# Exp and state update named at earlier steps of a software-pipelined retention, SoLU and cosine-MLP kernel

## The reference

```python
# retention over 4 batches, 8 heads, 768 positions, head size 64
state = gamma * state + k_t^T v_t          # 64 x 64 per head
y_t   = q_t @ state / 8
x     = y as (3072 tokens, 512)
# SoLU block, 512 -> 1024 -> 512
h    = x @ w_in
e    = exp(h - max(h));  sm = e / (sum(e) + 1e-9)
solu = h * sm
ln   = (solu - mean) / sqrt(var + 1e-6) * g_ln
x2   = ln @ w_out
# cosine block, 512 -> 2048 -> 512
h = x2 @ w_in2;  out = (h * cos(h)) @ w_out2
```

## Time and profile before

| | |
|---|---|
| median of 3 runs | 966.66 us |
| the profiled execution, device time | 966.66 us |
| its span, first to last instruction | 964.9 us |
| PE busy | 933.9 us (97%) |
| DVE busy | 732.9 us (76%) |
| ACT busy | 562.7 us (58%) |
| POOL busy | 266.0 us (28%) |
| DVE slices of 24 us up to 384 us | all 70% or more, most 90% or more |
| granted TensorE clock, whole span | 0.986 |

### The profile page before, as it was taken

One profiled execution on the slowest core, in us unless ns is written; L12 is line 12 of the kernel. 1 busy time (PEld: TensorE's weight loads), 2 busy tenths in 40 slices (PEclk: granted clock), 3 DMA queues, 4 the chain that ended last, 5 costly groups with the idle time before them and its releaser, 6 DMA issues.

```text
span 964.9 us, 14709 instructions
## 1 busy us (share of the span) xinstructions
PE 933.9 (97%) x4992; PEld 831.1 (86%) x4992; DVE 732.9 (76%) x1054; ACT 562.7 (58%) x922; POOL 266.0 (28%) x260
## 2 busy tenths in 40 slices
PE   3899999999999999999799999999999999999998
PEld 3688888888888888888699999999999999999997
DVE  7989899989999899976556677656775666765564
ACT  5656657657566566554555566546665556656453
POOL 2465576666665765731000000000000000000000
PEclk8799999999999999999899999999999999999999
DMA  7413454634653535435796544744345544364401
GB/s 276 153 66 115 147 204 137 217 110 145 221 178 132 193 137 189 154 98 164 280 316 194 141 117 123 230 139 120 111 129 179 180 110 129 111 192 114 117 12 65
DMA packets 106520, 148.18 MB, mean 154 GB/s; under 512 B 7408, under 2 KB 77040, under 8 KB 106480
## 3 DMA queue, kind: packets, MB, share of 16 engines
q1 hardware_dynamic: 106480, 147.69, 47.6%
HBM read 112.01 MB, written 35.65 MB: 153 GB/s over the span
## 4 chain that ended last, share of the span: by engine, by line
PE 79%; DVE 13%; issue 5%; ACT 2%; DMA 1%; POOL 0%; DVEq 0%; SPq 0%; ACTq 0%; POOLq 0%
PE bank L310 26%; PE bank L312 26%; PE bank L313 26%; DVE p_l L1065 2%; DVE q_l L1049 1%; PE bank L596 1%; DVE work L1115 1%; DVE p_m L1058 1%; DVE nmax L1109 1%; DVE x_l L1089 1%; DVE wo_out L1158 1%; DVE z_l L1142 1%; ACT x_h L749 1%; PE bank L619 1%; DVE work L1150 1%
## 5 line engine op out<-in xcount | busy, mean ns | idle before, releaser
L310 PE MATMUL bank<-yc_h,ring 128*128 128x384 f32 x448 | 152.3, 340 | 5.8 <-ACT e L872 2.5
L312 PE MATMUL bank<-yc_l,ring 128*128 128x384 f32 x448 | 152.2, 340 | 0.0
L313 PE MATMUL bank<-yc_h,ring 128*128 128x384 f32 x448 | 151.7, 339 | 0.0
L1185 DVE SCALAR_TENSOR_TENSOR gg<-turns,c 128x768 f32<-128x768 int32 x64 | 61.0, 953 | 65.2 <-ACT turns L816 65.2
L989 POOL TENSOR_TENSOR y_raw<-y_raw,t 128x768 f32<-128x768 f32 x4 | 7.4, 1854 | 367.9 <-DVE yc_l L1167 367.8
L816 ACT ACTIVATE turns<-c 128x768 int32<-128x768 f32 x64 | 54.2, 846 | 81.0 <-DVE c L1255 78.2
L822 ACT ACTIVATE gg<-gg 128x768 f32<-128x768 f32 x64 | 54.2, 847 | 80.0 <-DVE gg L1192 79.9
L310 PEld LDWEIGHTS bank<-yc_h,ring 128*128 128x128 f32 x448 | 84.7, 189 | 14.8 <-issue 7.4
L312 PEld LDWEIGHTS bank<-yc_l,ring 128*128 128x128 f32 x448 | 84.8, 189 | 7.1
L313 PEld LDWEIGHTS bank<-yc_h,ring 128*128 128x128 f32 x448 | 84.7, 189 | 0.0
L310 PE MATMUL bank<-w1i_h,x_h 128*128 128x512 f32 x192 | 80.1, 417 | 3.8 <-DVE x_l L1089 2.5
(11 more groups left out here) (129 smaller groups left out, 2489.5 us busy)
## 6 DMA issues: line engine op xcount, KB each, us to landing
ring<-w_split SPq DMA_DIRECT2D x224, 256.0 KB, 2.8
w_split<-w_out SPq DMA_DIRECT2D x16, 896.0 KB, 4.7
w2o_split<-wo_out SPq DMA_DIRECT2D x16, 512.0 KB, 4.1
w2o<-w2o_split SPq DMA_DIRECT2D x8, 1024.0 KB, 8.4
raw<-kT SPq DMA_DIRECT2D x24, 256.0 KB, 2.7
raw<-qT SPq DMA_DIRECT2D x24, 256.0 KB, 3.0
raw<-kn SPq DMA_DIRECT2D x24, 256.0 KB, 3.8
raw<-vn SPq DMA_DIRECT2D x24, 256.0 KB, 4.4
```

The source lines that it names most:

```text
L310: eng.matmul(dst, ah, bh, start=first and i == 0, stop=False, skip_group_check=read_between)
L312: eng.matmul(dst, ah, bl, start=False, stop=False, skip_group_check=read_between)
L313: m = eng.matmul(dst, al, bh, start=False, stop=last_one and i == n - 1, skip_group_check=read_between)
L1185: dve.scalar_tensor_tensor(gg[:, r, :], turns[:, r, :], -TWO_PI_HI, flat(c_32[:, r, :, :]), ALU.mult, ALU.add)\
```

## The change

The names `EX` and `ST` are taken out of the list. ACT's exp now stands under `L1b`, and DVE's state update stands under `DL`. PE's order and POOL's order stay as they are. ACT's order becomes T0, exp, T1, O0, SH, PQ, and DVE's becomes PL, L1b, state update, T1, O0, U. No instruction and no wait is added or removed. At position 1 the special list named `ST` right after `DL`, so there nothing moves. In the tail, the steps put in after `T1` now stand behind the exp, where they stood ahead of it.

```diff
 STEP = [("PK", 0), ("PV", 0), ("L1a", 2), ("SC", 1), ("WE", 1), ("T0", 3), ("PL", 1), ("L1b", 2),
-        ("DL", 1), ("T1", 3), ("EX", 2), ("ST", 1), ("WS", 0),
-        ("O0", 1), ("SH", 1), ("U", 2), ("PQ", 0), ("PN", 0),
+        ("DL", 1), ("T1", 3), ("WS", 0), ("O0", 1), ("SH", 1), ("U", 2), ("PQ", 0), ("PN", 0),
...
-                first = [("SC", 1), ("PK", 0), ("PL", 1), ("DL", 1), ("ST", 1), ("O0", 1), ("PV", 0),
-                         ("PQ", 0)]
+                first = [("SC", 1), ("PK", 0), ("PL", 1), ("DL", 1), ("O0", 1), ("PV", 0), ("PQ", 0)]
...
-                elif name == "EX":
+                elif name == "L1b":
                     wait(act, nm_done, b, t)
                     act.activation(e_b, ps_h[:, :, :].rearrange("p a n -> p (a n)"), ACT.Exp,
...
-                elif name == "ST" and c < TILES - 1:
+                elif name == "DL" and c < TILES - 1:
 
                     wait_state(dve, d_done, b, t)
                     wait_state(dve, sl_done, b, t - 1)
```

## The result

The changed kernel took 975.53 us (median of 4 runs, 975.04 to 978.78), the kernel before 966.75 us beside it. The ratio is 1.0098, with a 95% interval of 1.0076 to 1.0119: about 1% slower. The forecast was 977.8 us with a range of 973.5 to 982.

A forecast was written before the change was run, and what follows sets the result against it. PE, busy 97% and fed just in time by DVE, was taken as the bound. Loop 8.8 + 0.8 = 9.6 us, head 0.4 and tail 1.1 made 11.1 us on 966.66: 977.8 us, range 973.5 to 982.

The forecast's parts named there:

- Exp wins nothing, `z_h` is pushed behind it: On ACT in loop tiles: exp still waits for the row maximum; the second `z_h` starts at 269.23 instead of 265.90.
- 0.48 us per tile on DVE, 0.75 us of idle time ahead of `z_l`: DVE in ordinary tiles: 0.76 us idle ahead of `z_l` replaces 0.28 ahead of `x_l`; 0.48 us later, taken as 0.49.
- The state update covers part of the wait: On DVE, the 1.11 us state update runs while `z_l`, 1.86 us late, waits for `z_h`, leaving 0.76 us idle.
- PE: not 0.49 + 0.75, but DVE's pace: Ordinary tiles lose DVE's 0.49 us; PE's 0.75 us wait in L2a counts only at round starts, as 0.26 us more.
- the last rival: At the loop's `p_l` pair: a changed order against POOL's `k_l` makes the kernel faster, 964.8 us; chance 4%.
- one of the signs that the prediction named for being wrong: On DVE: the prediction is wrong if `p_l` or `q_l` change their durations.
- PE is fed just in time at O0: In an ordinary tile O0 starts 0.17 us after the `p_l` it needs, so DVE's delay reaches PE nearly whole.
- The tail, 1.1 us: At position 25: exp starts 0.20 us earlier, `z_h` and `z_l` come later, PE's L2a waits; 1.1 us lost.
- The head, 0.4 us: Exp comes behind a `z_h` in the head's last three tiles only: 0 to 1.5 us, taken as 0.4.
- The third block keeps the loss: After the tail, PE runs the third block in its own unchanged order, so the loss stays.
- a delay costs because DVE is the pace: In the loop DVE sets the pace, so its 0.49 us delay costs in each of 18 tiles, 8.8 us.
- The rule on the shared port: DVE beside POOL: `z_l` and the state update, one PSUM tensor each, run as before; the sum stays, `p_l` order open.

The follow-up runs named there:

- The doubled copy: The changed kernel with ACT making the second `z_h` copy of each tile twice, first into a spare buffer: 987.66 us, ratio 1.0220.
- the relieved kernels: Either order with DVE's `w2_out` low-part subtraction cut to 32 columns (before 965.16, changed 972.33 us) or both weight subtractions left out (963.98, 972.76 us).
- the kernel without the weights: The changed kernel without DVE's two subtractions for the third block's weights, whose low parts are zero: 972.76 us, ratio 1.0069.

## Why the prediction was right, point by point

**Exp wins nothing, `z_h` is pushed behind it.** Shown. Exp starts 0.04 us after the maximum in the kernel before and 0.03 us in the changed one; only its idle time ahead grew.

**0.48 us per tile on DVE, 0.75 us of idle time ahead of `z_l`.** Shown: 0.72 us idle, none ahead of `x_l`, `p_l` to `p_l` 18.44 us, which is 0.47 more. The doubled copy added 0.49 per tile.

**The state update covers part of the wait.** Shown by the exp moved alone, 28 us slower instead of 10, and by the state update moved alone, no change.

**PE: not 0.49 + 0.75, but DVE's pace.** In ordinary tiles the addition was right: tiles 4 and 5 of the second round grew by 0.47 and 0.49 us. The loop grew by 8.79 us, forecast 9.6, and the rounds by 2.88, 2.83 and 3.08 us. That 6 x 0.49 = 2.9 covers this nearly is in part luck, for two things at the start of a round cancel. The first tile grew by 1.00 us, more than the forecast 0.49 + 0.26. The second did not grow at all (-0.06 us), because DVE's pair of `p_l` got shorter there, in the kernel before and in the changed one:

```profile
228.31 2.64 DVE L1065 TENSOR_TENSOR p_l<-p_m,p_h 128x512 fp32r<-128x512 f32 x2
```

```profile
233.37 2.16 DVE L1063 TENSOR_TENSOR p_l<-p_m,p_h 128x512 fp32r<-128x512 f32 x2
```

It starts 1.58 us after POOL's `k_l` instead of 1.12. In the other two rounds the pair went from 2.63 to 2.15 and from 2.47 to 2.15 us. This is the mechanism of the last rival, in one tile of six, and a changed `p_l` is one of the signs that the prediction named for being wrong. Without it the loop would have grown by some 10 us, an estimate: 8.79 + 0.48 + 0.48 + 0.32.

**PE is fed just in time at O0.** This reading was not right. The 0.17 us between `p_l` and O0 is no wait on record: O0 follows the transposes in PE's queue. What tied PE to DVE in the ordinary tile before was `x_l` (0.26 us of the weight load, at 275.87), and in the changed kernel it is `z_l` in L2a.

**The tail, 1.1 us.** 0.98 us were measured. `z_l` came at 452.30, after a wait of 1.75 us, and PE waited 0.74 us by the record, 0.9 by the spacing of its matmuls.

**The head, 0.4 us.** 1.25 us were measured in the one profile, but the same stretch lies between 104.8 and 107.3 us in the relieved kernels, in either order, so this term isn't settled.

**The third block keeps the loss.** The loss was kept but for 1 us that goes with the granted clock of that execution.

The median came out 2.3 us below the forecast. Of this the loop explains 0.8 us and the third block 1.0; the profiled execution was itself 1.2 us above the median; the head went 0.85 us the other way.

**What was wrong in the reasons** is the sentence that a delay costs because DVE is the pace. For an ordinary tile of the changed kernel it holds, and the trace settles it: DVE waits there for nothing but `z_h`. The path over PE has room, from `p_m` to the end of `z_l` 294.51 - 285.23 = 9.28 us and an estimate of 8.46 us for PE's part, taken from the kernel without the weights: 17.74 us, below DVE's 18.44. But the sentence did not say what would lift the cost. With two subtractions per tile taken from DVE, 6.0 of the 8.8 us in the loop stayed. They stayed in other tiles: at the start of a round, and in the fifth tile, where the path from PE's scores through ACT, DVE and a `p_l` slowed to 3.27 us back to L2a takes 18.50 us, above PE's 17.89. The loss in the ordinary tiles vanished when the part that all these chains share got shorter, at `p_l`.

**The rule on the shared port.** The Trainium skill, "SBUF — State Buffer", section "Who interferes with whom", lets a DVE instruction with at most one SBUF input run beside GpSimd. The trace agrees: `z_l` took 0.68 us beside POOL's `k_l` (at 287.71) and 0.69 us where POOL was idle for most of it (at 293.82), and the state update 1.11 us wherever it came. What the rule leaves open, the order at `p_l`, did shift: not in the ordinary tiles (2.63 us for the pair), but in the second tile of each round, in the good direction, and in the kernel without the weights in the bad one (3.27 us).

## What to carry to other kernels

When two instructions in an in-order queue are swapped, ask which of their inputs is there first: the one whose input is already there belongs ahead, in the other's idle time. In this kernel the copy was free there, and behind the exp it cost 0.47 to 0.49 us in an ordinary tile. Then count the cost on the engine whose queue waits at the end of the chain, and don't add PE's waits on top of it. Taking work from the busiest engine may cure some tiles only, while another path of nearly the same length goes through it in the others; look at every tile of a round and not at one, and for the piece that the paths share.

## What was not expected of the hardware

A DVE subtraction with two SBUF inputs, cut from 512 to 32 columns, still took 0.87 us instead of 1.36 us, as POOL's instruction beside it ran until just before its end. With all 512 columns it took 0.87 us too in the second tile of a round of the changed kernel, where DVE came to it later. And `p_l` for 512 columns took between 0.68 us and 1.8 us in these runs. That this depends on what POOL does is shown by one run: shortening POOL's `k_l` and `v_l` to 32 columns, which took POOL 0.70 us each, made DVE's pair 0.83 us shorter.
